# A fused attention and two-MoE kernel: local normalisation moved to VectorE, the sum over v split between two engines, and the loads around the pooled v reordered

## The reference, cut to what matters

```python
def _attn_ref(q, k, v):                       # (4, 8, 576, 64)
    q_d = q.reshape(B, H, Sd, factor, D).mean(axis=3)   # factor 4, Sd = 144
    k_d = k.reshape(B, H, Sd, factor, D).mean(axis=3)
    v_d = v.reshape(B, H, Sd, factor, D).mean(axis=3)
    out_up = np.repeat(sm_attn(q_d, k_d, v_d), factor, axis=2)
    mask = np.abs(pos[:, None] - pos[None, :]) < factor # a band of 7
    scores = np.where(mask, scale * np.matmul(q, k.transpose(0, 1, 3, 2)), -1e9)
    attn = softmax(scores)
    return out_up + np.matmul(attn, v)
def _moe_ref(x, w_a, w_b, w_out):             # 2304 tokens, 512 -> 1536 -> 512
    return (x @ w_a) * (x @ w_b) @ w_out
def _moe2_ref(x, w_in, w_out, g_ln):          # 512 -> 1024 -> 512
    h = x @ w_in
    solu = h * softmax(h)
    return layernorm(solu) * g_ln @ w_out
```

## Time and profile before

| what | us |
|---|---|
| median of 3 runs | 793.88 |
| lowest and highest of them | 793.29, 794.19 |
| the profiled execution's own time | 792.38 |
| its span in the trace | 790.6 |
| TensorE busy | 757.9 (96% of the span) |
| VectorE busy | 561.8 (71%) |
| ScalarE busy | 298.9 (38%) |
| GpSimd busy | 212.6 (27%) |

### The profile page before, as it was taken

How to read it: one execution, slowest core, us unless ns; L and a number is a source line. 1 busy time by engine, 2 the same in 40 slices (tenths; PEclk the granted TensorE clock), 3 DMA queues, 4 the chain that set the end, 5 groups by cost and what they waited for, 6 DMA issues and landing times.

```text
span 790.6 us, 12316 instructions
## 1 busy us (share of the span) xinstructions
PE 757.9 (96%) x4464; PEld 695.8 (88%) x4464; DVE 561.8 (71%) x975; ACT 298.9 (38%) x819; POOL 212.6 (27%) x260
## 2 busy tenths in 40 slices
PE   7678899798999999999999999999999999999998
PEld 7567889798999999999999999999988888888886
DVE  4479999979878887878777876022477666666663
ACT  3534656254253525354524434224322222222222
POOL 2468897546313421051001112121100000000000
PEclk9669999999999999999999999999999999999999
DMA  9999968494888586683946433637121011011011
GB/s 189 204 242 230 201 144 264 158 308 113 267 220 248 174 244 185 186 220 90 259 160 195 153 97 110 210 100 229 36 67 53 27 54 54 27 55 54 28 40 41
DMA packets 96652, 117.27 MB, mean 148 GB/s; under 512 B 19921, under 2 KB 59603, under 8 KB 96593
## 3 DMA queue, kind: packets, MB, share of 16 engines
q1 hardware_dynamic: 81872, 106.98, 48.6%
q10 hardware_dynamic: 14721, 9.51, 4.2%
HBM read 95.62 MB, written 20.84 MB: 147 GB/s over the span
## 4 chain that ended last, share of the span: by engine, by line
PE 80%; issue 0%; ACT 0%
PE psum L862 25%; PE psum L864 24%; PE psum L863 24%; PE psum L974 2%; PE psum L818 1%; PE psum L798 1%; PE psum L808 1%; PE psum L829 1%; PE psum L780 0%; ACT out_sb L1273 0%; ACT out_d L1088 0%
## 5 line engine op out<-in xcount | busy, mean ns | idle before, releaser
L862 PE MATMUL psum<-x_hi,w_hi 128*128 128x384 f32 x576 | 199.2, 346 | 1.1 <-DVE x_lo L1386 1.1
L864 PE MATMUL psum<-x_hi,w_lo 128*128 128x384 f32 x576 | 194.3, 337 | 0.0
L863 PE MATMUL psum<-x_lo,w_hi 128*128 128x384 f32 x576 | 194.2, 337 | 0.0
L862 PEld LDWEIGHTS psum<-x_hi,w_hi 128*128 128x128 f32 x576 | 109.2, 190 | 4.2 <-issue 3.6
L863 PEld LDWEIGHTS psum<-x_lo,w_hi 128*128 128x128 f32 x576 | 109.3, 190 | 0.0
L864 PEld LDWEIGHTS psum<-x_hi,w_lo 128*128 128x128 f32 x576 | 109.2, 190 | 0.0
L1392 DVE TENSOR_TENSOR ab_f<-psum,a_sb 128x384 f32<-128x384 f32 x72 | 39.9, 554 | 91.7 <-PE psum L864 63.4
L862 PE MATMUL psum<-ab_hi,wo_hi 128*128 128x384 f32 x288 | 100.4, 349 | 3.9 <-issue 3.7
L864 PE MATMUL psum<-ab_hi,wo_lo 128*128 128x384 f32 x288 | 97.1, 337 | 0.0
L863 PE MATMUL psum<-ab_lo,wo_hi 128*128 128x384 f32 x288 | 97.0, 337 | 0.0
L1700 POOL TENSOR_TENSOR raw<-raw 96x256 f32<-96x256 f32 x60 | 57.3, 981 | 129.1 <-DMA raw<-in_q 59.9
(11 more groups left out here) (149 smaller groups left out, 1416.0 us busy)
## 6 DMA issues: line engine op xcount, KB each, us to landing
wo_hi<-wo_hi_scratch SPq DMA_DIRECT2D x53, 256.0 KB, 2.8
wo_lo<-wo_lo_scratch SPq DMA_DIRECT2D x53, 256.0 KB, 3.1
k_u<-in_k SPq DMA_DIRECT2D x11, 576.0 KB
v_u<-in_v SPq DMA_DIRECT2D x11, 576.0 KB
k_u<-in_k SPq DMA_DIRECT2D x17, 288.0 KB
v_u<-in_v SPq DMA_DIRECT2D x17, 288.0 KB
wo_raw<-in_moe_w_out SPq DMA_DIRECT2D x19, 256.0 KB, 2.9
raw<-in_v SPq DMA_DIRECT2D x8, 576.0 KB, 7.6
```

Source lines behind the costliest of these rows:

```text
L862: mm(dst, wh, xh, start=first, stop=False, skip_group_check=not check)
L863: mm(dst, wh, xl, start=False, stop=False, skip_group_check=not check)
L864: last = mm(dst, wl, xh, start=False, stop=end, skip_group_check=not check)
```

## The change

Six edits, all in the head:

1. The multiplication of `p_loc` by the inverse goes from GpSimd (`normalise`, four times) to the end of VectorE's `head_inverse`.
2. The sums of the second half of the first batch's v go from GpSimd (`pool_rows(0, 2, 1)`, six instructions) to VectorE (`head_v_sums`, two instructions, after `head_mask(3)`). A semaphore `raw_by_vector` is added, and `store_vd(0, 1)` waits on it.
3. SP loads `q_u` (`load_unit_q(1, 0)`, four DMAs) between the two stores.
4. SP loads `k_u` (`load_unit_k(1, 0)`, four DMAs) after `load_vd(0)`, which stands directly behind the second store.
5. The first `w_out` block (`load_wo(0)`) is loaded before the first store.
6. `keep_busy` before `head_scores(0)` and `head_scores(1)` makes two matmuls instead of three.

```diff
--- before.py
+++ after.py
@@ -334,8 +334,8 @@
 
 
 
-    POOL_SUMS = [(b, tau, half) for b, taus in ((0, (2,)), (1, (2, 0, 1)), (2, (2, 0, 1)), (3, (2, 1, 0)))
-                 for tau in taus for half in range(2)]
+    POOL_SUMS = [(0, 2, 0)] + [(b, tau, half) for b, taus in ((1, (2, 0, 1)), (2, (2, 0, 1)), (3, (2, 1, 0)))
+                               for tau in taus for half in range(2)]
 
     RAW_PASS = [(1, 2), (1, 1), (2, 2), (2, 0), (2, 1), (3, 2), (3, 1)]
 
@@ -366,7 +366,7 @@
         h_turned qT_by_vector qT_by_scalar kT_ready kd_ready qd_summed qd_ready h_scored h_masked h_exped h_inv_ready h_normed h_p_turned h_pT_ready h_x_mm
         hp_scored hp_bias_ready hp_exped hp_normed hp_turned hp_pT_ready
         h_up_mm x_local x_summed
-        raw_by_pool raw_step qk_turned qk_out pool_scored pool_bias_ready pool_exped pool_inv_ready
+        raw_by_vector raw_by_pool raw_step qk_turned qk_out pool_scored pool_bias_ready pool_exped pool_inv_ready
         p_turned pT_out out_mm_d out_d_ready
         loc_chain k_used v_used q_used u_sub_ready u_exped u_normed u_act_values acc_ready x_turned x_hi_ready x_lo_ready
         w_hi_ready w_lo_by_vector w_lo_by_pool wo_hi_ready wo_lo_by_vector wo_lo_by_pool
@@ -458,7 +458,10 @@
 
             def store_vd(b, half):
                 t, _, _ = raw_buffer(b, 2, half)
-                sp.wait_ge(s.raw_by_pool, raw_by_pool(b, 2, half))
+                if (b, half) == (0, 1):
+                    sp.wait_ge(s.raw_by_vector, 1)
+                else:
+                    sp.wait_ge(s.raw_by_pool, raw_by_pool(b, 2, half))
                 sp.dma_start(vd_dram[b].rearrange("(p s) e -> p s e", s=6)[:, 3 * half:3 * half + 3, :],
                              t[:, 0, :, 128:256]).then_inc(vd_stored[half], 16)
 
@@ -532,14 +535,14 @@
             load_raw(0, 2, 0)
             load_raw(0, 2, 1)
             load_weights(0)
+            load_wo(0)
+            store_vd(0, 0)
             load_unit_q(1, 0)
-            load_unit_k(1, 0)
-            store_vd(0, 0)
             store_vd(0, 1)
             load_vd(0)
+            load_unit_k(1, 0)
             load_raw(1, 2, 0)
             load_raw(1, 2, 1)
-            load_wo(0)
             load_wo(1)
             load_weights(1)
             load_raw(1, 0, 0)
@@ -697,7 +700,7 @@
             def head_scores(c):
                 at_least(pe, s.h_masked, c)
                 if c < 2:
-                    keep_busy(bank(2), 3)
+                    keep_busy(bank(2), 2)
                 wait_qT(c)
                 pe.wait_ge(s.kT_ready, c + 1)
                 par = c % 2
@@ -1325,6 +1328,18 @@
                 chain.link(V.tensor_scalar(loc_den[:, c % 2, :], loc_sum[:, c % 2, :], 1e-9, None, ALU.add))
                 at_least(dve, s.h_normed, c - 1)
                 V.reciprocal(loc_inv[:, c % 2, :], loc_den[:, c % 2, :]).then_inc(s.h_inv_ready, 1)
+                dve.wait_ge(s.h_inv_ready, c + 1)
+                p = p_loc[:, c % 2]
+                V.tensor_tensor(p, p, loc_inv[:, c % 2, :].unsqueeze(2).to_broadcast([2 * QR, LT, WIN]), ALU.mult
+                                ).then_inc(s.h_normed, 1)
+
+            def head_v_sums():
+
+                t, loaded, count = raw_buffer(0, 2, 1)
+                dve.wait_ge(loaded, count)
+                chain.link(V.tensor_tensor(t[:, :, :, 0:128], t[:, :, :, 0:128], t[:, :, :, 128:256], ALU.add))
+                V.tensor_tensor(t[:, 0, :, 128:256].rearrange("p s (x d) -> p x s d", x=2),
+                                t[:, :, :, 0:D], t[:, :, :, D:2 * D], ALU.add).then_inc(s.raw_by_vector, 1)
 
             def both(first, second, count):
 
@@ -1537,6 +1552,7 @@
             head_scale()
             head_inverse(2)
             head_mask(3)
+            head_v_sums()
             head_local(1)
             head_pooled_max(0)
             head_pooled_max(1)
@@ -1686,12 +1702,6 @@
             G.affine_select(out=edge[:, 2], in_=edge[:, 2], compare_op=ALU.is_ge, fill=MASKED,
                             base=NT - 1 + PAD, pattern=behind, channel_multiplier=-TPP).then_inc(s.edge_ready, 1)
 
-            def normalise(c):
-                pool.wait_ge(s.h_inv_ready, c + 1)
-                p = p_loc[:, c % 2]
-                G.tensor_tensor(p, p, loc_inv[:, c % 2, :].unsqueeze(2).to_broadcast([2 * QR, LT, WIN]), ALU.mult
-                                ).then_inc(s.h_normed, 1)
-
             def pool_rows(b, tau, half):
                 t, loaded, count = raw_buffer(b, tau, half)
                 pool.wait_ge(loaded, count)
@@ -1726,12 +1736,7 @@
                 G.tensor_tensor(ab_lo[:, g % 2, :], ab_f[:, g % 2, :], ab_hi[:, g % 2, :], ALU.subtract
                                 ).then_inc(s.ab_lo_by_pool, 1)
 
-            normalise(0)
-            normalise(1)
             pool_rows(0, 2, 0)
-            pool_rows(0, 2, 1)
-            normalise(2)
-            normalise(3)
             for tau in (2, 0):
 
                 if tau == 2:
```

## The result

The changed kernel takes **797.63 us** (median of 12 runs, 795.62 to 800.71), beside 794.01 for the kernel before on the same chip: a ratio of 1.0049, interval 1.0030 to 1.0068. It is slower by 0.5%, 3.9 us, where 4.0 us of gain were forecast. The profiled execution took 797.33 us with a span of 795.5, against 792.38 and 790.6.

The account below looks back on a forecast made before the run. The head's chain of waits, decided by the load of `v_d`, was taken as the bound, then VectorE in the first tile. That load's 4.0 us gain, other terms zero, gave 793.88 - 4.0 = 789.9 us; range 786.9 to 794.3.

Parts of the forecast that it names:

- The whole kernel is as late as the end of that chain: Head: a chain of waits up to the first `up_product` at 51.07 us decides when the whole kernel ends.
- the balance: Second batch's q: 3.8 us more loads ahead, stream restarting 4.0 us sooner, so GpSimd reaches weight block 2 near 64.
- Two passes less ... zero at the end: Shorter `keep_busy` in the head: first scores 0 to 0.5 us sooner, lost in the DMA wait, zero at the end.
- The price of VectorE's new work: Head: four multiplications of 0.58 us and 1.5 us for the sums over v, 3.8 us in all.
- The `v_d` chain: Head: load of `v_d` issued at 32.8 instead of 36.81, `head_up(0)` at 36.9, 4.0 us sooner.
- Block 2: First tile: TensorE's matmul waits nearly 4 us for GpSimd's weights, made up by a later 2.87 us wait going away.
- VectorE's work sets the pace: First tile after block 2: VectorE, busy 92.3 of 93 us, starts 4.0 us sooner, so the tile ends 4.0 sooner.
- The gain drowns in block 2: Rival, first tile: GpSimd's low part late or VectorE not past its product, no gain, 793.9 us; chance 0.20.
- More than the 4.0: Rival, head: TensorE's clock stays high from 38 to 51 us, 3 us more gain, 786.9 us; chance 0.10.
- The load of `v_d` doesn't come sooner: Rival, head: first store holds back `q_u` and second store, load after 33.0, up to 3.8 us more, 797.7; chance 0.05.
- New starvation as priced: Rival, first tile: GpSimd's weights starve two more VectorE instructions, 4.2 us each, 798.3 us; chance 0.08.
- a loss of at most one GpSimd instruction: Shared SBUF port: by the skill's rule a contending VectorE instruction would lose at most 0.7 us; the trace showed 4.2.

Follow-up runs that it names:

- e1_keep3: The changed kernel with `keep_busy` back at three matmuls before `head_scores(0)` and `head_scores(1)`; 798.69 us, ratio 1.0063.
- e2_old_loads: The changed kernel with SyncE's load order of the kernel before, the work moved to VectorE kept; 794.81 us, ratio 1.0008.
- e9_both_links: The changed kernel with `k_u` behind the second batch's raw v, and w_out's block 3 ahead of w_in's block 3 and raw k; 793.42 us.
- e6_wo3_first: The changed kernel with the load of w_out's block 3 ahead of w_in's block 3 and raw k; 795.53 us, ratio 1.0028.
- e4_weights_first: The changed kernel with GpSimd making the low parts of weight and w_out block 2 before its second-batch q sums; 798.40 us, ratio 1.0061.

## Why the prediction was wrong

*"The whole kernel is as late as the end of that chain": wrong, and the first failure.* I read the earlier trace rows as one chain of waits ending at the first `up_product`. e1_keep3 has that row at 46.84 and loses 0.6%; e2_old_loads has it at 51.96 and loses nothing. In the changed kernel the first tile follows the loads that come after `v_d` instead: with `k_u` behind raw v and w_out's block 3 issued sooner, the engine work unchanged, the 0.49% is gone (e9_both_links). That it passes through GpSimd's sums and ScalarE's high parts is read from the waits, not tested by itself.

*"0.92 MB more ... 3.8 us; but the stream restarts 4.0 us sooner. So GpSimd still reaches weight block 2 at about 64": the balance failed.* In the changed kernel the stream restarts at 34.01 against 36.81, 2.8 us sooner, but it runs dry 5 us sooner (the share is 0.63 in the first microsecond from 30 on and 0.32 in the next, against 0.31 from 35 to 36 before). I had moved both ends by the same 4.0 us; here the hole widens. But that is not where the forecast broke. In e1_keep3 both ends moved by about 4 us, as I had it, and GpSimd still reaches weight block 2 at 67.93, against 68.11 in the changed kernel and "still near 64" in the forecast. Raw v reaches it at 45.69 and raw q at 58.29 there, against 43.30 and 54.47 before: 2.4 and 3.8 us later, where my balance gave about nothing for q. Part of it is the rate: from 38 to 58 us it is 224 GB/s in the changed kernel and 225 in e1_keep3, against 242 before, where I used 244. Over 20 us that is 0.34 MB, 1.5 us by my estimate. The rest stays open.

*"Two passes less ... zero at the end": the mechanism was missed.* The scores of pair 1 take 2.29 us at 14.40 with two matmuls and 1.29 at 14.04 with three (e1_keep3), the next pair's likewise (2.29 at 20.13, 1.29 at 18.16), and the sums over v slip from 26.49 to 30.36. That put the second store at 31.94 instead of the forecast 29.4. It is true, but not for my reason, that this is worth nothing at the end: with three matmuls the time is 798.69.

*The price of VectorE's new work: right.* Sums 0.95 + 0.56 = 1.51 us (forecast 1.5), multiplications 0.59 (0.58). Only their start was late.

*The `v_d` chain: nearly right.* Load at 34.01 (forecast 32.8; 33.02 in e1_keep3), `head_up(0)` at 38.61 (36.9; 37.45), first `up_product` at 48.02 (47.1; 46.84).

*Block 2: only half seen.* I forecast a wait of nearly 4 us at a block 2 that starts near 65.6; it starts at 69.56 after 4.82. I then asked only whether the next wait would swallow it. The queue behind was not looked at: w_out's block 3 is issued behind raw k, which waits for the stores of the second batch, and lands later with them. Its correction alone (e6_wo3_first) is 0.21 of the 0.51 points that e9_both_links takes back, with the uncertainty said above.

*"VectorE's work sets the pace", 4.0 us sooner: wrong here.* From 60 to 100 us it is busy 19.36 + 17.00 = 36.4 of 40 us, against 39.7 before, so it is no longer full. That its input came from the late batch is argued and not shown: in e9_both_links it is busy only 34.8 us of these 40, and nothing is lost. A busy time that contains starved instructions doesn't say how much work was done.

*The rivals.* "The gain drowns in block 2" had 0.20 and 793.9. Its condition held (GpSimd's low part came at 68.11 and TensorE waited for it), but its price left out that the batch itself could come later than before, and it was 3.7 us too low. "More than the 4.0" didn't happen: the granted clock from 38 to 51 us is 0.50, as before. "The load of `v_d` doesn't come sooner" had 0.05 and a price of 797.7. Its condition (after 33.0) held, its effect ("`k_u` only delays the second batch") was real, and its number fits, by luck in part, since it was worked out for a load that comes no sooner at all. Its trigger didn't hold: the first store wasn't what held the second, and e1_keep3 loses as much with the load at 33.02. It should not have hung on that threshold. New starvation as priced, two more instructions, did not happen: between 56 and 100 us the long VectorE rows are 6.12, 5.63 (for two) and 4.08 us in the changed kernel, and 5.14, 4.42 and 3.96 before. That starvation has a part in the loss isn't excluded, since e9_both_links has the 6.12 alone. As to the rule of the Trainium skill, "SBUF — State Buffer", section "SBUF: two separate sides", that whoever starts first holds the shared port pair for the whole instruction: I had read it as a loss of at most one GpSimd instruction, and the trace disagrees on the size again. The VectorE instruction from 68.62 to 74.74 outlasts GpSimd's four at 68.11, two at 70.85 and most of four at 72.22.

## What to carry to other kernels

When loads are moved behind a store and its read-back, count what remains queued to cover the round trip (here that hole cost nothing measurable once `k_u` stood behind raw v), and follow the bytes that were moved to whoever is now behind them, down to loads that wait for another event on the same queue. Here a head that was 4.2 us shorter was worth nothing while the first tile's data came later, so test a claim on the path by a kernel that makes the head shorter and leaves the loads alone. And a wait at one place, once removed, may only show the next: e4_weights_first removed 4.8 us of waiting and gained nothing. Check a meter (a wait, a start, a busy share) on a variant that loses nothing before you trust it: three of those used here failed that.
